# The attention's weighted sum by query halves instead of by key blocks, its rows three wide products a head

## What is computed

```
B, H, S, D = 2, 8, 768, 64;  E = 8 experts;  N = B*S = 1536 tokens, DM = H*D = 512
q_bucket, k_bucket = 6 sign bits of q @ proj and k @ proj
scores = (q @ k.T) / 8 where the buckets agree, else -1e9
attn   = exp(scores - max) / (sum + 1e-9)
x      = attn @ v, rows of all heads side by side        # [1536, 512]
logits = x @ w_gate                                       # [1536, 8]
each token goes to its best expert that has room (192 places each), by order of logits
x = relu(x[mask] @ w1[e]) @ w2[e]
h = x @ w_in;  out = (h * sigmoid(h)) @ w_out
```

## Time and profile before

| | us |
|---|---|
| median of three runs | 855.26 |
| lowest, highest | 854.28, 857.5 |
| the profiled execution, its time | 852.95 |
| its span, first to last instruction | 851.2 |
| attention | from 12 to 301 |
| routing and experts | to 560 |

### The profile page before, as it was taken

One profiled execution on the slowest core, in us unless ns is written; L12 is line 12 of the kernel. 1 busy time (PEld: TensorE's weight loads), 2 busy tenths in 40 slices (PEclk: granted clock), 3 DMA queues, 4 the chain that ended last, 5 costly groups with the idle time before them and its releaser, 6 DMA issues.

```text
span 851.2 us, 14868 instructions
## 1 busy us (share of the span) xinstructions
PE 793.9 (93%) x5504; PEld 649.9 (76%) x5504; DVE 523.0 (61%) x1241; ACT 274.1 (32%) x592; POOL 99.7 (12%) x144
## 2 busy tenths in 40 slices
PE   6999999999999943999999998999999999999996
PEld 4677777676767633899899997998888788878885
DVE  5887788877888689596797784264333433333331
ACT  3566666666666510122211211232110311130111
POOL 4111221312223301010011010000000100010001
PEclk9999999999999975799999999999999999999999
DMA  6114415053250206065155146640000100010001
GB/s 131 39 38 109 97 38 126 20 124 84 52 126 10 78 20 222 2 224 195 42 211 213 60 176 223 259 163 1 1 1 0 50 0 0 0 49 0 0 0 49
DMA packets 74602, 68.78 MB, mean 81 GB/s; under 512 B 52288, under 2 KB 60480, under 8 KB 73536
## 3 DMA queue, kind: packets, MB, share of 16 engines
q1 hardware_dynamic: 70976, 60.82, 23.8%
q0 software_dynamic: 2240, 7.34, 2.4%
q10 hardware_dynamic: 1344, 0.04, 0.1%
HBM read 61.90 MB, written 6.29 MB: 80 GB/s over the span
## 4 chain that ended last, share of the span: by engine, by line
PE 82%; DVE 9%; DMA 5%; issue 2%; ACT 1%; POOL 1%; SPq 0%; ACTq 0%; DVEq 0%; POOLq 0%
PE pt_ps L1326 15%; PE score_ps L1309 15%; PE pt_ps L1232 9%; PE pt_ps L1134 8%; PE pt_ps L1242 6%; PE score_ps L1106 4%; PE pv_ps L1106 4%; PE score_ps L1090 4%; PE score_ps L1091 4%; DMA area<-x_rows,ids_now 4%; PE work_ps L1179 2%; DVE area L955 2%; DVE area L898 1%; PE work_ps L1062 1%; PE score_ps L1062 1%
## 5 line engine op out<-in xcount | busy, mean ns | idle before, releaser
L1326 PE MATMUL pt_ps<-y_s,w_in_s 128*128 128x512 f32 x576 | 137.8, 390 | 2.7 <-DVE y_s L1017 2.0
L1309 PE MATMUL score_ps<-w_out_s,gate_s 128*128 128x512 f32 x576 | 137.4, 389 | 0.0
L1326 PEld LDWEIGHTS pt_ps<-y_s,w_in_s 128*128 128x128 f32 x576 | 107.9, 188 | 26.1 <-DVE y_s L1017 2.8
L1309 PEld LDWEIGHTS score_ps<-w_out_s,gate_s 128*128 128x128 f32 x576 | 108.1, 188 | 22.4
L1035 DVE TENSOR_TENSOR gate<-pt_ps,sig 128x512 f32<-128x512 f32 x48 | 33.2, 692 | 146.4 <-ACT sig L597 146.4
L483 ACT ACTIVATE att_area<-att_area 128x768 f32<-128x768 f32 x96 | 90.0, 937 | 87.9 <-DVE att_area L793 87.8
L793 DVE TENSOR_SCALAR_CACHE_REDUCE att_area<-score_ps 128x768 f32<-128x768 f32 x96 | 91.7, 955 | 21.0 <-PE score_ps L1091 19.6
L1232 PE MATMUL pt_ps<-area,experts_w 128*128 128x192 f32 x512 | 98.7, 341 | 2.9 <-ACT area L557 2.9
L597 ACT ACTIVATE sig<-pt_ps 128x512 f32<-128x512 f32 x48 | 28.7, 598 | 210.5 <-PE pt_ps L1326 210.5
L1242 PE MATMUL pt_ps<-area,experts_w 128*128 128x192 f32 x512 | 89.0, 329 | 1.3 <-ACT area L561 1.3
L1232 PEld LDWEIGHTS pt_ps<-area,experts_w 128*128 128x128 f32 x512 | 84.1, 194 | 3.9 <-ACT area L557 3.9
(11 more groups left out here) (190 smaller groups left out, 935.7 us busy)
## 6 DMA issues: line engine op xcount, KB each, us to landing
experts_w<-in_moe_w SPq DMA_DIRECT2D x16, 2048.0 KB, 9.1
experts_w<-in_k SPq DMA_DIRECT2D x16, 384.0 KB, 4.8
experts_w<-in_q SPq DMA_DIRECT2D x16, 384.0 KB, 5.5
experts_w<-in_moe_w_in SPq DMA_DIRECT2D x8, 512.0 KB, 4.8
w_out_raw<-in_moe_w_out SPq DMA_DIRECT2D x4, 1024.0 KB, 8.9
att_area<-in_v SPq DMA_DIRECT2D x16, 192.0 KB, 2.3
x_rows<-att_area SPq DMA_DIRECT2D x8, 384.0 KB, 3.5
area<-x_rows,ids_now POOLq DMA_INDIRECT x16, 5.4
```

What stands on the lines that cost most here:

```text
L1309: done = nc.tensor.matmul(out_ps[m], gate_s[:, fo % RING_S, a, m * P:(m + 1) * P], w_out_s[:, fo, b, :], start=(fo == 0 and a + b == 0), s ...
L1326: done = nc.tensor.matmul(layer_ps[f % 2][:, 0:GT], w_in_s[:, a, w_cols], y_s[:, c, b, :], start=(c == 0 and a + b == 0), stop=(c == DC - ...
```

## The change

In the weighted sum the two column groups now hold the two query halves of the same key block. A pair is one key block, six pairs make a head, and all of them are done in the units of the next head, where `weighted(h, p, b, loads)` has unit b = t. The bank then holds the finished sum over all keys, the first query half in the upper and the second in the lower partitions. ScalarE copies a head in one op, before unit 0. The turned probabilities get two buffers a head half, one pair of them in a free part of `experts_w`, so that a head's can be filled while the last one's are read.

The rows are three products: the stationary tile holds query block t of one half above block t of the other, and `to_x` is a whole 128x128 identity and twice the gate's columns, each with zeros in the other's half, 128 + 16 = 144 columns. They are done two heads behind (`fill_work("x", ..., h - 2)`), so in the opening pair there are none and two lots come after the last head: one between the second and third of six pairs, one at the end. The logits of that last stretch come first on VectorE, and the last x is divided after `find_best`.

```diff
-    DE = D + E
+    DE = 2 * (D + E)
+    TH = T // 2
...
-        probs_t = [att(T, HALF).rearrange("p b (t q) -> p b t q", t=3) for _ in range(2)]
-        weighted_t = att(S)
+        weighted_t = [att(HALF) for _ in range(2)]
...
+        probs_t = [[att(T, HALF) for _ in range(2)], [expert_w(4 * T * P + s * T * HALF, 0, T * HALF).rearrange("p (b n) -> p b n", b=T) for s in range(2)]]
...
-            if not opening:
-                e[(4, 0)] = ("x", 0, len(e), 1)
+            if not first:
+                e[(4, 0)] = ("x", 0, len(e), 2)
...  SyncE
-                    if p == 0 and write:
-                        sp.wait_ge(s_work_free, x_drained(g))
-                        sp.dma_start(x_out(g - 1), x_nat).then_inc(s_xw, 16)
-                for p in range(2):
-                    h = 2 * g + p
-                    sp.wait_ge(s_pv, 2 * h + 2)
-                    load_v(h + 2, p)
+                if write:
+                    sp.wait_ge(s_pv, 2 * g)
+                    load_v(2 * g + 1, 1)
+                    sp.wait_ge(s_work_free, x_drained(g))
+                    sp.dma_start(x_out(g - 1), x_nat).then_inc(s_xw, 16)
+                sp.wait_ge(s_pv, 2 * g + 1)
+                load_v(2 * g + 2, 0)
...  ScalarE
-                nc.scalar.activation(weighted_t[:, ch * HALF:(ch + 1) * HALF], pv_banks[ch][:, 0:HALF], ACT.Copy).then_inc(s_turned, 1)
+                nc.scalar.activation(weighted_t[p], pv_banks[p][:, 0:HALF], ACT.Copy).then_inc(s_turned, 1)
...  GpSimd
+            nc.gpsimd.memset(to_x[:, :, P:DE], 0.0).then_inc(s_gate_zero, 1)
...
-                for r0 in (0, D):
-                    step(nc.gpsimd.tensor_copy(to_x[r0:r0 + D, :, 0:D],
-                                               ident[r0:r0 + D, r0:r0 + D].unsqueeze(1).broadcast_to([D, H, D])))
+                step(nc.gpsimd.tensor_copy(to_x[:, :, 0:P], ident[:, :].unsqueeze(1).broadcast_to([P, H, P])))
...  VectorE
+            def over_rows(bank, a, b):
+
+                rows = bank[:, 0:TH * DE].rearrange("p (t e) -> p t e", e=DE)
+                return rows[:, :, a:b].rearrange("p t (s e) -> p t s e", s=2)
...
+            def logits_of(p, bank):
+
+                nc.vector.tensor_tensor(head_logits.rearrange("p (s t) e -> p t s e", s=2), over_rows(bank, P, DE),
+                                        inv_of(p, E), ALU.mult).then_inc(s_head_logits, 1)
+
+            def x_of(p, bank):
+
+                cols = x_nat[:, :, p * D:(p + 1) * D].rearrange("p (s t) d -> p t s d", s=2)
+                nc.vector.tensor_tensor(cols, over_rows(bank, 0, P), inv_of(p, D), ALU.mult).then_inc(s_work_free, 1)
...
+                    if not first:
+                        dve.wait_ge(s_head_logits, h - 1)
+                        dve.wait_ge(s_work_free, w if last else w - 1)
...
-            drain_work("x", 0, W_LAST, 0, None, bank=LAST_BANK)
...
+            for p in range(2):
+                dve.wait_ge(s_work_full, W_LAST + p + 1)
+                dve.wait_ge(s_logits, HEADS - 1 + p)
+                logits_of(p, work_banks[p])
+                dve.wait_ge(s_head_logits, HEADS - 1 + p)
+                nc.vector.tensor_tensor(last_part, last_part, head_logits, ALU.add).then_inc(s_logits, 1)
+                if p == 0:
+                    dve.wait_ge(s_xw, 16 * PAIRS)
+                    x_of(p, work_banks[p])
...
             find_best(0)
+            x_of(1, work_banks[1])
             find_wants(0)
...  TensorE
-                    for t in range(T):
-                        if t % 3 == 0:
-                            pe.wait_ge(s_turned, 2 * h + 1 + t // 3)
-                        last = nc.tensor.matmul(bank[:, t * DE:(t + 1) * DE], weighted_t[:, t * P:(t + 1) * P], rhs,
+                    pe.wait_ge(s_turned, h + 1)
+                    for t in range(TH):
+                        last = nc.tensor.matmul(bank[:, t * DE:(t + 1) * DE], weighted_t[p_next][:, t * P:(t + 1) * P], rhs,
...
-                for b in (2 * u, 2 * u + 1):
-                    r0 = D * (b % 2)
-                    done = nc.tensor.matmul(pv_banks[ch][r0:r0 + D, 0:HALF], v_nat[p][:, b, :],
-                                            probs_t[ch][:, b, :, :].rearrange("p t q -> p (t q)"),
-                                            start=(u == 0), stop=(u == 2))
+                for half in range(2):
+                    done = nc.tensor.matmul(pv_banks[p][half * D:(half + 1) * D, 0:HALF], v_nat[p][:, b, :],
+                                            probs_t[p][half][:, b, :, :].rearrange("p t q -> p (t q)"),
+                                            start=(b == 0), stop=(b == T - 1))
...
-            for u in range(3):
-                weighted(2 * HEADS - 1, 1, 1, u, 0)
-            fill_work("x", 0, W_LAST - 1, HEADS - 1, 0, 0, LAST_BANK)
+            for b in range(T):
+                weighted(HEADS - 1, 1, b, PAIRS - 1)
+                if b == 1:
+                    fill_work("x", 0, W_LAST - 1, HEADS - 2, 0, 0, work_banks[0])
+            fill_work("x", 0, W_LAST, HEADS - 1, 1, 0, work_banks[1])
```

## The result

| | before | after |
|---|---|---|
| median of four runs each, us | 854.77 | 844.82 |
| lowest, highest | 854.27, 857.5 | 844.05, 848.23 |
| profiled execution, its time | 852.95 | 844.72 |
| its span | 851.2 | 843.0 |

The ratio is 0.988, 95% interval 0.985 to 0.9915: 1.2% faster, 10.0 us against 7.2 forecast. Against the 848.1 us that were forecast it is 3.3 us less: 2.8 of effect, and 0.5 because the fourth run put the median before at 854.77. The 90 executions of the kernel before that were timed beside the later experiments have a median of 855.1, all ten of the changed one 844.7.

The account below looks back on a forecast made before the run. TensorE bounds the steady heads. Rows -7.8, head 0 -0.95, head 1 -1.35 and tail +2.9 sum to -7.2 us, so 848.1 us against the median 855.26; the 8-in-10 range is 845.0 to 853.0.

Parts of the forecast that it names:

- The rows in a steady head: Heads 2 to 15: six 144-column records at 0.123 us replace twelve of 72; 0.56 us saved a head, 7.8 us.
- Rival 1: The rows' weight loads are exposed, 0.233 us a record, losing 0.1 us a head; 858.6 us, chance 0.04.
- Rival 3: VectorE paces more: head 0 gives nothing, steady heads only half of 0.56 us; 852.9 us, chance 0.13.
- The pairs: The weighted sum's 96 pairs, now one key block of both query halves, keep their 0.80 us; costed at nothing.
- Rivals 2 and 4: Sharing a v block makes pairs slower, 856 to 863 us, chance 0.06; or faster, toward 0.65 us, 841 us, chance 0.03.
- Heads 0 and 1: Half a head's pairs leave head 0, saving 0.95 us; the rows leave head 1, saving 1.35 us.
- The tail: After the last head: three added pairs, the rows of head 14, and waiting for one ScalarE copy; +2.9 us.
- SyncE's order: Loads of q and k precede the write of x; v loads stop waiting for the next head's third unit; costed nothing.
- What is behind the attention: Routing, experts and last layer hang on the chain and move up with it; no further gain or loss.
- The clock: Half clock between attention and first expert: each microsecond of later rise costs about half; 2 us allowed both ways.

Follow-up runs that it names:

- rows72: The changed kernel with each wide product of the rows cut in two of 72 columns, twelve records a head again: 855.25 us, ratio 1.000.
- tail_late: The changed kernel with the rows of head 14 behind all six pairs of the tail instead of behind the second: 846.39 us, ratio 0.990.
- v_behind: The kernel before with the changed kernel's SyncE order, the odd head's v loaded behind the next pair's q and k: 854.08 us, ratio 0.998.
- the pads: One-column products added at TensorE's start to move instruction fetches: 18 in the changed kernel, 845.26 us (0.989); 46 in the one before, 854.63 us (0.998).
- ctl_before: The kernel before run once more without an edit, for a second profile: 853.95 us, ratio 1.000.
- pairs_33: The changed kernel with the pairs of units 4 and 5 both done in unit 3, behind its own: 840.22 us, ratio 0.983.
- pairs_33t: The changed kernel with the edits of pairs_33 and tail_late together: 839.91 us, ratio 0.982.
- pad_before: The kernel before with 46 one-column f32 products at TensorE's start, so its fetches fall where the changed kernel's do: 854.63 us, ratio 0.998.
- ctl_after: The changed kernel run once more without an edit, for a second profile: 844.43 us, ratio 0.988.

## Why the prediction was right in kind and short in size

**The rows in a steady head.** Right to 0.01 us: spacing 0.123, 0.83 from the first record to the pair, 0.56 saved a head, 7.9 us in fourteen. rows72 gave all of it back. Rival 1 fell with it: loads of 0.19 us each stood behind records spaced at 0.123. Its price of 0.1 us a head was not what its own terms give (five times 0.233 and 0.20 are 1.37, against 1.38 before: nothing), which changed nothing in the forecast. Rival 3 fell too, as steady heads gave all of the 0.56.

The sentence of the Trainium skill that the forecast weighed ("TensorE: Matmul & The Clock Gate", Part 3, "The mechanism": a load overlaps only where the row group differs) would have had the loads exposed; the measurement decides against it here. The same section also lets a load go ahead into a background weight buffer, and 0.123 us a record fits that.

**The pairs.** At nothing, right: the medians of their records are 512 and 486 ns in both kernels. Rivals 2 and 4 didn't occur.

**Heads 0 and 1.** The sum had -0.95 and -1.35, together -2.3. Units 3 to 5 of head 0 gave 1.22 us (9.95 to 8.73), more than the step said; 0.27 of it came from unit 3, whose pair the forecast had called hidden. Head 1 gave 0.97: its unit 4 became 2.63, not 2.24 like unit 3. VectorE, at work there without a pause since 39.88, had read the block before only at 47.11, and TensorE's scores start at 47.26. Together -2.2: two misses that cancel.

**The tail.** +3.1 against +2.9. tail_late shows that 0.92 of it was the order: the rows of head 14 in the middle of the pairs cost two changes of shape and left ScalarE's copy bare.

**SyncE's order: the first step that failed.** That the loads of q and k go ahead of the write of x, and that the loads of v no longer wait as they did, was costed at nothing, since no load was on the path in the steady heads that I read. In the kernel before k was late in some heads (two of them in its first profile, 4 and 12, with 18.04 and 18.19 us instead of 17.89), because v was loaded ahead of it (v_behind). Worth 0.5 to 0.9 us. A mean head should have been taken from all fourteen, not from head 2.

**What is behind the attention: the second.** That all behind it hangs on the chain and moves up with it is false for TensorE's instruction fetch. Its place goes with the number of TensorE's instructions (the pads moved it), the gather's with the work; the change moved one against the other, and the first gathered block came 2.2 and 1.2 us sooner after the issue in the two pairs of profiles (1.7 in the mean of the six profiles against the ten). The rows of before don't show it; that a fetch fell into the gather's 7.4 us could have been read from the trace of before, and what the change would do to it could not.

**Whether it adds up.** First profiles: -7.9 (rows), -2.2 (heads 0 and 1), +3.1 (tail), -0.5 (k) and -2.2 (fetch) are -9.7. The opening took back 2.4 and the experts gave 0.9, which makes -8.2, the measured difference of the spans. Second profiles: -7.9, -2.2, +3.1, -0.9 and -1.2 are -9.1. The opening took back 0.7, ctl_before had two short stretches at half clock, 0.8 and 1.7 us, and the experts took back 0.5: -10.4, of 10.7 measured. So the change itself is worth some 9.1 to 9.7 us in these profiles, against 7.2 forecast.

**The clock.** The prediction allowed 2 us either way, and gave the whole allowance to one place, the rise at 350. There the changed kernel spent 37.5 us at half clock and the one before 41.0, in ctl_before 3.4 and 37.5. Its price, about half a microsecond for each that the rise comes later than the work, was right: over the 14 profiles whose second gather is not the long one, the time from the first gathered block to the second expert's first gather is 25.1 us and 0.45 for each us from that block to the rise (27.35 at 4.9 us in pairs_33, 28.82 at 8.1 in before), none more than 0.05 off. That makes 0.5 us of the experts' 0.9 in the first pair of profiles, and the 0.5 that they took back in the second.

But other places move as much. One is the opening. The clock rose at 12.0 us in the first profile of the kernel before, at 18.3 in ctl_before, at 20.6 and 20.4 in the two of the changed one. Head 0's first two units take 5.47 to 5.48 us in the four profiles where they have the full clock throughout (before, rows72, pairs_33, pairs_33t), 5.8 in the three where it rises 1.4 to 1.6 us after head 0 starts, and 6.3 to 6.4 in the nine where that is 2.7 us or more (v_behind and pad_before, which have the old rows, among them). So the time of the opening goes with its clock, and a late rise comes in either kernel. Another is the experts. The table by stretch of an expert in ctl_before, then in ctl_after:

```profile
522.00:540.00 18.00, 15.37 (x103) 14.49 (x103) 3.77 (x23) 2.97 (x8) 1.89 (x2) 0.91 0.46 179
```

```profile
522.00:540.00 18.00, 16.44 (x120) 15.68 (x121) 5.00 (x27) 3.86 (x11) 1.89 (x2) 1.00 0.58 212
```

In ctl_before a stretch of 3.4 us at half clock, a spell, began at 533.7 us, and the expert in which it fell took 21.65 us from gather to gather instead of 19.91. There was none in either profile of the changed kernel nor in the first of the one before, and there was one in ten of the sixteen profiles, rows72, tail_late and v_behind among them.

Over the 90 executions of the kernel before, the time goes with the mean granted clock (which doesn't count the opening): 852.7 us is the median of the 29 at 0.974 or more, 858.9 that of the 22 at 0.969 or less; the correlation of time and microseconds at half clock is 0.80, and each of these goes with 0.42 us. The first profile of before, 852.95 at 0.974, is such an upper one, and the changed kernel's, 844.72 at 0.976, too. Between executions at 0.974 or more the medians are 852.7 (29) and 844.05 (5), 8.7 us apart; between all of them, 855.1 (90) and 844.7 (10), it is 10.4. The median execution of the kernel before had 47.8 us at half clock, the changed kernel's 45.5, worth 1.0 by that slope. That the change makes for more of the high clock isn't shown; ten executions are few.

So of the 2.8 us that the forecast lacked, the two steps costed at nothing are worth 2.1 to 2.7 by the profiles. Up to 1.0 more can be the clock's mix, by luck of the executions timed. The timing, with an interval of 7.3 to 12.8 us, can't divide it further.

## What to carry to other kernels

- Where a record costs the same at 72 and at 128 columns, halve the number of f32 products by widening them: 144 columns cost 0.123 us a record and 72 cost 0.112. Then try where the other pieces of work stand: moving one pair by a unit gave half as much again (17.33 to 17.03 a head), and moving three by a unit lost 6 us.
- Read the waits of all turns of a loop before taking one as the mean, and when the order on a DMA queue changes, look at what its waits were holding back.
- Compare profiles only at the same granted clock, the opening's too; here 6 us between executions of one kernel went with it, more than most edits gave.

## What the runs showed of the hardware that I had not expected

- TensorE's code is fetched in 16 KB pieces while it runs. One of them 4 to 5 us behind a gather's issue held up the gather's own landing: 7.0 us to the first block in the mean of six profiles, against 5.2 in ten, and 5.31 to 6.62 when nothing but the fetch was moved.
- An indirect DMA's instruction on GpSimd took 1.01 us in 14 profiled executions and 7.26 in two, the same code among both.
- The records of one core's granted clock show spells of 3.4 us (once 6.8) at half clock inside dense work (522 to 540 us, TensorE busy for 85% of it), which come and go between executions of the same kernel. Where there was one, in ten of sixteen profiles, it began 181 to 184 us behind the rise in the first expert.
- What that rise costs was steady: 0.45 us for each us that it came later behind the first gathered block, to 0.05 us over 14 profiles.
